# Reordering the opening and the last tiles of a fused linear-attention and two-expert kernel on one core

## The reference

```python
for t in range(S):                                   # attention, per batch and head
    cur = (u * k_t) outer v_t
    y_t = r_t @ (state + cur)
    state = w_t[:, None] * state + k_t outer v_t
x = y, heads side by side                            # 3072 tokens x 384
h = x @ w_in                                         # first expert, 384 -> 1024
solu = h * softmax(h); ln = (solu - mean) / sqrt(var + 1e-6) * g_ln
x = ln @ w_out                                       # 1024 -> 384
h = x @ w_in2; out = maximum(0.01 * h, h) @ w_out2   # second expert, 384 -> 2048 -> 384
```

## Time and profile before

| what | value |
|---|---|
| median of 3 runs | 788.29 us (788.03 to 789.04) |
| the profiled execution's own time | 792.25 us |
| its span, first to last instruction | 790.1 us |
| mean granted TensorE clock | 0.997 of full |
| PE / DVE / ACT / POOL busy | 99 / 66 / 43 / 23% of the span |
| DMA | 45.89 MB, 58 GB/s over the span |

### The profile page before, as it was taken

One profiled execution on the slowest core, in us unless ns is written; L12 is line 12 of the kernel. 1 busy time (PEld: TensorE's weight loads), 2 busy tenths in 40 slices (PEclk: granted clock), 3 DMA queues, 4 the chain that ended last, 5 costly groups with the idle time before them and its releaser, 6 DMA issues.

```text
span 790.1 us, 12141 instructions
## 1 busy us (share of the span) xinstructions
PE 779.6 (99%) x4638; PEld 735.4 (93%) x4638; DVE 517.6 (66%) x1020; ACT 341.5 (43%) x676; POOL 179.5 (23%) x203
## 2 busy tenths in 40 slices
PE   8999999999999999999999999999999999999997
PEld 4779999999999999999999999999999999999997
DVE  7787999966666676657747567485674765553432
ACT  4468554534334353443434443344443434334332
POOL 4751413330222212212212123022120230100000
PEclk9999999999999999999999999999999999999999
DMA  9960122122113021020120310202202111000001
GB/s 256 314 214 6 62 66 66 32 64 66 36 31 96 1 66 44 23 95 6 61 66 1 96 46 21 66 18 79 66 1 66 44 53 31 1 1 31 0 1 35
DMA packets 19666, 45.89 MB, mean 58 GB/s; under 512 B 1952, under 2 KB 14752, under 8 KB 19216
## 3 DMA queue, kind: packets, MB, share of 16 engines
q1 hardware_dynamic: 15952, 37.17, 15.6%
q10 hardware_dynamic: 3648, 7.87, 3.1%
HBM read 40.31 MB, written 4.72 MB: 57 GB/s over the span
## 4 chain that ended last, share of the span: by engine, by line
PE 80%; DVE 1%; issue 0%; ACT 0%; DVEq 0%
PE BANKS L1187 56%; PE MISC L1187 20%; PE BANKS L1366 2%; PE MISC L1211 1%; PE MISC L1204 1%; DVE ki L873 0%; DVE W2L L1021 0%; DVE att L863 0%; DVE A L886 0%; DVE Rraw L1005 0%; DVE RL L1012 0%; DVE X2L L1027 0%; ACT X2H L744 0%; ACT OUT L750 0%; DVE diag L893 0%
## 5 line engine op out<-in xcount | busy, mean ns | idle before, releaser
L1187 PE MATMUL BANKS<-RH,W4H 128*128 128x384 f32 x384 | 135.4, 353 | 0.0
L1187 PE MATMUL BANKS<-X2H,W3H 128*128 128x384 f32 x384 | 130.8, 341 | 0.2 <-DVE X2L L1027 0.2
L1187 PE MATMUL BANKS<-X2L,W3H 128*128 128x384 f32 x384 | 129.4, 337 | 0.0
L1187 PE MATMUL BANKS<-RH,W4L 128*128 128x384 f32 x384 | 129.2, 336 | 0.0
L1187 PE MATMUL BANKS<-X2H,W3L 128*128 128x384 f32 x384 | 129.2, 336 | 0.0
L1187 PE MATMUL BANKS<-RL,W4H 128*128 128x384 f32 x384 | 129.0, 336 | 0.0
L1005 DVE TENSOR_TENSOR Rraw<-BANKS,Rraw 128x384 f32<-128x384 f32 x128 | 70.7, 552 | 86.7 <-ACT Rraw L723 85.7
L723 ACT ACTIVATE Rraw<-BANKS 128x384 f32<-128x384 f32 x128 | 62.6, 489 | 136.5 <-PE BANKS L1187 136.3
L727 ACT ACTIVATE RH<-Rraw 128x384 fp32r<-128x384 f32 x128 | 67.1, 524 | 101.5 <-DVE Rraw L1005 101.5
L873 DVE RECIPROCAL ki<-att 112x128 f32<-112x128 f32 x96 | 89.5, 938 | 0.0
L1012 DVE TENSOR_TENSOR RL<-Rraw,RH 128x384 fp32r<-128x384 f32 x128 | 71.7, 560 | 22.5 <-ACT RH L727 22.5
(11 more groups left out here) (141 smaller groups left out, 1500.7 us busy)
## 6 DMA issues: line engine op xcount, KB each, us to landing
att<-rkw SPq DMA_DIRECT2D x23, 672.0 KB, 4.8
rtok<-r_tok SPq DMA_DIRECT2D x22, 192.0 KB, 2.6
ktok<-k_tok SPq DMA_DIRECT2D x22, 192.0 KB, 2.7
vtok<-v_tok SPq DMA_DIRECT2D x22, 192.0 KB, 3.4
out<-OUT SPq DMA_DIRECT2D x7, 576.0 KB, 4.3
W3raw<-w_in ACTq DMA_DIRECT2D x1, 3072.0 KB, 20.5
W4raw<-w_out ACTq DMA_DIRECT2D x1, 3072.0 KB, 13.5
W1raw<-w_in SPq DMA_DIRECT2D x2, 768.0 KB, 12.1
```

The source lines that it names most:

```text
L1187: return nc.tensor.matmul(dst, lhsT, rhs, start=start, stop=stop, skip_group_check=True)
```

## The change

1. SP: the decays of chunk 1 get a transfer and a semaphore of their own, as chunk 0's have. The order of issue becomes: chunk 0, decays of chunk 1, u, tokens of chunk 0, r and k of chunk 1, then as before. DVE's `decay(0, 1)` waits for the decays alone; `undecayed_keys` and POOL's `decayed_queries` of the first three chunks wait for the rest.
2. POOL: in chunk 0 the own-token products stand ahead of `end_keys`.
3. DVE: `own_sums(0, 0)` stands ahead of the first reciprocal of chunk 1, and `row_max(0, 0)` ahead of the third masks.
4. PE: one `unread` goes; the second half of `first_expert(0)` stands ahead of the scores of chunk 2.
5. PE: the last nine groups of three matmuls go in the order DRAIN, pairs of (output, tile).

```diff
+DRAIN = ((0, 0), (0, 1), (1, 0), (1, 1), (2, 0), (0, 2), (1, 2), (2, 1), (2, 2))
...
+            def load_decay(m):
+                sp.dma_start(att[:, m, 2, :, :].rearrange("p a t -> p (a t)"),
+                             rkw[m * PD:(m + 1) * PD, 2 * PAIRS * CH:3 * PAIRS * CH]).then_inc(ld_decay[m], 16)
...
-                if first(b, m) and m == 0:
-                    sp.dma_start(to[:, 2, :, :].rearrange("p a t -> p (a t)"),
-                                 rkw[0:PD, 2 * PAIRS * CH:3 * PAIRS * CH]).then_inc(ld_decay, 16)
+                if first(b, m) and m < 2:
+                    if m == 0:
+                        load_decay(0)
                     both, part = slice(0, 2), slice(0, 2 * PAIRS * CH)
...
             load_T(0, 0)
+            load_decay(1)
+            sp.dma_start(ub[:, :], u.partition_broadcast(CH)).then_inc(ld_u, 16)
+            load_tok(0, 0)
             load_T(0, 1)
-            load_tok(0, 0)
-            sp.dma_start(ub[:, :], u.partition_broadcast(CH)).then_inc(ld_u, 16)
...
             def decayed_queries(b, m):
+                if first(b, m):
+                    wait_T(pool, b, m)
...
             decayed_queries(0, 0)
-            end_keys(0, 0)
             pool.wait_ge(ld_u, 16)
             own_token(0, 0, 0)
+            end_keys(0, 0)
             own_token(0, 0, 1)
...
             def decay(b, m):
-                if first(b, m) and m == 0:
-                    dve.wait_ge(ld_decay, 16)
+                if first(b, m) and m < 2:
+                    dve.wait_ge(ld_decay[m], 16)
...
             def undecayed_keys(b, m, portion=(0, PAIRS)):
                 a, n = portion
+                if first(b, m):
+                    wait_T(dve, b, m)
...
             mask(0, 0, 2)
-            inverse(0, 1, 0)
             own_sums(0, 0)
-            inverse(0, 1, 1)
+            for a in (0, 1):
+                inverse(0, 1, a)
...
             take_state(0, 1)
+            row_max(0, 0)
             for a in (0, 2):
                 mask(0, 2, a)
             own_sums(0, 2)
-            row_max(0, 0)
...
-            def cons(b, kind, so, f, fp):
+            def cons(b, kind, so, f, fp, outs=range(KM)):
...
-                for m in range(KM):
+                for m in outs:
...
-                last.then_inc(pe_cons, 1)
+                if KM - 1 in outs:
+                    last.then_inc(pe_cons, 1)
...
-                    if len(waiting) > 2:
+                    by_output = closing(b, kind, so) and f == F2 - 1
+                    if len(waiting) > 2 and not by_output:
                         cons(b, *waiting.pop(0))
...
+                    if by_output:
+                        for m, i in DRAIN:
+                            cons(b, *waiting[i], (m,))
+                        waiting = []
...
             first_state(0)
-            unread(1)
             first_transposes(0)
...
             first_state(1)
+            first_expert(0, (1,))
             first_scores(2)
-            first_expert(0, (1,))
             first_transposes(1)
```

More of the change, by code:

```diff
@@ L255, in build @@
         consts, chain = sem("consts"), sem("chain")
-        ld_decay, ld_w1a, filled = sem("ld_decay"), sem("ld_w1a"), sem("filled")
+        ld_decay = [sem("ld_decay0"), sem("ld_decay1")]
+        ld_w1a, filled = sem("ld_w1a"), sem("filled")
         split_hi = [sem(f"split_hi{i}") for i in range(4)]
```

## The result

| | before | changed |
|---|---|---|
| median, 20 runs each | 788.39 us | 791.96 us |
| lowest to highest | 786.46 to 793.44 us | 789.92 to 797.2 us |
| profiled execution, own time / span | 792.25 / 790.1 us | 790.98 / 788.9 us |
| mean granted clock in the profiled one | 0.997 | 1.0 |

The ratio is 1.0036 [1.002, 1.0052]: the changed kernel is slower by about 2.8 us, and the forecast of 787.5 us was wrong. (Ratios compare mean times of runs of one call, a run over 1.5% above the fastest of its kernel left out, so they differ somewhat from what two medians give.) The two profiled executions mislead by themselves: that of the changed kernel is 1.0 us under its own median and one of only three in twenty with a mean clock of 1.0, and that of before is 3.9 over its median. So what follows rests on more than this pair.

A forecast was written before the change was run, and what follows sets the result against it. TensorE was taken as the bound, busy 779.6 of 790.1 us, so gains come only at the ends. Head 0.4 plus tail 0.4 made 0.8 us won: 787.5 us forecast (profiled 791.4), range 785.2 to 790.0.

The forecast's parts named there:

- SP's queue: Load issue order at the start: tokens and u taken to land at 10.4 us, first expert 0.5 us sooner.
- T3: Chunk 3's 672 KB transfer, awaited by DVE's decays: landing taken 0.4 us sooner, at 41.2, so first_out(0) at 48.6.
- With tokens at 11.84: Bad bound in the head: end_keys ends at 15.0, 2.0 after PE wants it; first expert starts 1.0 us later.
- rival (b): Clock falls in a 2.2 to 2.6 us hole before first_out(0), losing 1.7: 790.0, or 789.6 with tail; chance 0.17.
- Case (c): The forecast case: chunk 3's transfer within 0.6 us of before, no clock fall, 786.8 to 788.5 us; chance 0.47.
- The bytes up to there are the same: SP's queue: later loads go out some 0.45 us later with unchanged bytes ahead of them.
- rival (a): Chunk 3's transfer lands by 39.2 us, W3 not later: 2.4 won, 2.8 with tail, 785.5 us; chance 0.36.
- The removed unread pair: PE at 15.10 to 16.15 us, beside take_y: removing it costs and gives nothing more.
- The expert half and row_max: Third scores at full clock, 1.73 us; chunk 1 transposes at 29.5 not 32.74, 3.2 us sooner.
- 0.4 won out of 3.2: Head: of 3.2 us gained by PE, only 0.4 survives the wait for chunk 3's transfer before first_out(0).
- W3 gates X(2): ACT waits for W3, landing at 39.75: X of chunk 2 ready at 41.1, third pass 2.2 us sooner, 1.0 given back.
- Tail: Last nine matmul groups reordered: last-landing store gains 0 to 0.5 us, 0.4 taken; 0.1 at risk.

The follow-up runs named there:

- e15_u_last: Kernel before with chunk 1's decays as their own transfer and tokens ahead of the rest of chunk 1, u still behind it: 788.41 us, ratio 0.9981.
- e5_sp_only: Kernel before with only SP's new order, the split decays and their waits; POOL and DVE keep their orders: 797.69 us, ratio 1.0107.
- e2_queue: Kernel before with SP's new order, split decays, own-token products ahead of end_keys, and own_sums ahead of the reciprocals: 792.59 us, ratio 1.0022.
- e6_pool_only: Kernel before with only own-token products ahead of end_keys and own_sums ahead of the reciprocals, SP as before: 792.87 us, ratio 1.0029.
- e9_changed: The changed kernel, unedited, run once more for a second profile: 792.23 us, ratio 1.0023 to before.
- e4_same: The kernel before, unedited, run again under its own name: 789.03 us, ratio 0.9974.
- e10_w3_later: e7_keys_first with ACT's issue of W3 moved behind take_keys(0, 1): 789.7 us, ratio 0.9994 to before.
- e16_keys_t3_first: e7_keys_first with chunk 3's transfer issued ahead of chunk 4's: 789.16 us, ratio 1.0022 to before.
- e7_keys_first: The changed kernel with end_keys(0, 0) put back ahead of the own-token products: 796.52 us, ratio 1.0091 to before.
- e3_drain: Kernel before with only the last nine groups of matmuls in the order DRAIN: 787.8 us, ratio 0.9964.
- e8_fill_hole: The changed kernel with one and a half unread matmul pairs put ahead of the first key transposes: 797.54 us, ratio 1.0093 to before.
- e12_expert_drain: Kernel before with the first expert's second half ahead of the third scores, row_max first, and DRAIN: 787.66 us, ratio 0.9976.
- e13_t3_first: Kernel before with chunk 3's transfer issued ahead of chunk 4's: 788.27 us, ratio 0.9986.
- e14_best: e12_expert_drain with chunk 3's transfer issued ahead of chunk 4's: 786.57 us, ratio 0.9961 to before.
- e17_pool_fill: e6_pool_only with one and a half unread matmul pairs ahead of the first key transposes: 789.99 us, ratio 1.0025 to before.

## Why the prediction was wrong

In short: two steps on SP's queue and one on POOL failed. The tokens landed later than I took them, the hole that this opened on PE can drop the clock, and the queue falls so far behind that T3 comes late whenever the hole does not. Either way first_out(0) comes late. Two numbers support this. Behind first_out(0) both profiles of the changed kernel take 739.2 us (788.9-49.67 and 790.1-50.86), so what differs between them lies ahead of it. And the changed kernel's three runs at a mean clock of 1.0 have 789.92 to 790.98 us, the fifteen at 0.993 to 0.996 have a median of 792.02: the fall costs some 1.2 us here, and without it the kernel is still 1.5 to 2.6 over before's median.

**SP's queue: "I bound their landing by 9.0 and 11.84 and take the middle, 10.4". This step failed.** POOL's own-token product, which waits for all three tokens, started at 11.37 behind vtok: 1.0 later than forecast. The issues weren't the cause: u's took 0.43 us and not 1.13, so vtok went out at 3.62 and not 4.3. The transfers behind u were slower: vtok landed 7.6 us after its issue. u's early place is the cause: e15_u_last differs from e5_sp_only in it alone, and its vtok takes 4.9 us for 7.8. Why this spread of one row over 128 partitions is slow was not tried.

**POOL: the bound was stated, its consequence was not.** "With tokens at 11.84 ... the first expert starts 1.0 later than before" counted the hole at its own length. The profile of the changed kernel shows that: a hole of 1.79 and the first expert at 17.78, 0.4 later. But the second profile, e2_queue's and e6_pool_only's have the granted clock at 0.50 from 15 us on, after holes of 1.95, 1.58 and 1.31, and in e9_changed it is still 0.50 in the whole window to 25 us. I had named this mechanism, rival (b), with the row that shows it (0.92 us of idling and 0.50 behind it), but I looked for it only at 49 us, and had just made a longer hole among narrow matmuls at 13 us by my own bound. Case (c) then said of late tokens "the T3 gate hides it too". In e9_changed it doesn't: PE is so late that T3 is in time, and PE itself is the bound, at 50.86. Of the changed kernel's 20 runs 15 have a mean granted clock of 0.993 to 0.996, so the falling clock is its rule and the first profile the exception. How much is lost can only be estimated, since both profiles of before are over its median. A run's time is some 2.1 us over its span, and from first_out(0) to the end it is 739.7 us in e4_same (787.3-47.62) and 739.2 in the changed kernel. By this estimate before's median of 788.39 has first_out(0) near 46.6 and the changed kernel's 791.96 near 50.6: 4 us lost in the head, 0.5 won behind it. The medians are 3.6 apart, the means 2.8.

**SP's queue again: "The bytes up to there are the same", so T3 only slides by 0.4. Wrong in size and sign, but masked.** The bytes are the same, the time that they take is not: 4.40 MB by 19 us with u in front, 5.52 with it behind (e5_sp_only, e15_u_last), a backlog that the prediction put at nothing. In e5_sp_only, where no hole delays ACT, T3 takes 17.5 us instead of 13.9. The remedies show that it is W3 and T4 competing with it: W3 later (e10_w3_later, ratio 0.9994) or T3 ahead of T4 (e16_keys_t3_first, 1.0022 and three runs of twelve still at 796 or more) where e7_keys_first has 1.0091. This is the mirror of rival (a), which I had named in one sentence and given no price. Had the head gone as I forecast, this would probably have been the result: e7_keys_first is 4 us slower than the changed kernel. The Trainium skill's page "DMA: Bandwidth & Descriptors", section "Queues, rings and completion order", has a DMA engine turn from one queue to the next only after a whole packet. From this the prediction had drawn that T3's landing might jump by microseconds, and it does: the same T3 takes 10.0 us with W3 later and 17.5 in e7_keys_first, which has W3 in its old place. Whether the packets' alternation is the reason, no run here shows.

**"The removed unread pair ... costs and gives nothing": only while POOL is late.** In three profiles with `end_keys` first it leaves 1.37, 1.72 and 1.48 us of idling ahead of the first transposes (e7, e10, e16), and in e7 and e10 the first expert's six matmuls then took 4.39 and 4.54 us instead of 2.84. In the changed kernel the later key work covers it.

**T3 gates first_out(0) by 7.41 us: right.** From the decays' start to first_out(0), where the decays waited for T3, it is 7.40 in the changed kernel (42.27 to 49.67), e4_same, e3_drain, e5_sp_only and e8_fill_hole, 7.39 in e7_keys_first and 7.41 in e12_expert_drain. With the expert half moved the gate is loose below about 37.3: there PE arrives last, at 45.1.

**The expert half and row_max: right.** 1.89 us for 1.89, and no clock fall at 27 us. 3.2 us were forecast at the transposes and 2.3 came, the difference being the head's own delay (17.78 where 16.85 was forecast: 0.9). "0.4 won out of 3.2" holds for it as long as T3 is late; with T3 in time the same edit is worth the step from e13_t3_first's 788.27 to e14_best's 786.57, 1.7 us with DRAIN in it. But of the 3.2 the 1.7 of clock belonged to the one profile that I summed against. Of the eight profiles that keep the third scores first and have a hole of 0.4 to 0.9 us there, only before's and e13_t3_first's show the fall. Against e4_same's 30.85 the changed kernel's 30.42 is 0.4 sooner, not 2.3.

**W3 gates X(2): right.** 41.71 was its copy and 42.23 the third pass, where 41.1 was forecast; W3 landed 1.2 later than I had it (40.96 for 39.75).

**Tail: 0.4 forecast, 0.6 by the medians of the profiles**, not separable by times. That the store which landed last (4.4 us) would gain fits the profiles: with DRAIN none of ten ends is long.

**Sum.** Head 0.4 won: in fact some 4 lost, by the estimate above. The range's upper end, 790.0, was set by rival (b) at 49 us alone; a second place for the same mechanism, with the 1.0 of the bound and a fall over a few microseconds of narrow matmuls, would have put it beyond 792. A slip besides: in rival (a) half of the 2.8 us gives 786.9, not 786.6; the forecast's own sum doesn't use it.

## What to carry to other kernels

When an unknown landing is bounded from both sides, follow the bad bound to its last consequence: a hole on TensorE among narrow matmuls is to be priced with a possible fall of the clock and not at its length alone. Holes of 0.92 us and more had it here in some executions, and it went with 4.8 us in e6_pool_only and some 1.2 in the changed kernel, where T3's gate hides the rest. Look at several executions before summing against one: the profile of before had both a fallen clock and a late T3, which its repetition lacked. Before moving a transfer forward, list which large loads of another engine's queue are then issued sooner, and which small late loads they get ahead of. When one remedy makes a change worse, look for a second loss that the first one was hiding, and undo both.

## What was unexpected of the hardware

- The clock's fall is a matter of chance at the same instructions: of two profiles of the changed kernel, the hole of 1.79 us was followed by 1.00 throughout and that of 1.95 us by 0.50 until at least 25 us. Of two of the kernel before, each with a hole of 0.92 us at 26 us, one fell to 0.50 and one stayed at 1.00. Of e6_pool_only's twelve runs three have a mean clock of 1.0.
- Unread matmuls put into the hole kept the clock at 1.00 in both profiles that have them (e17_pool_fill, e8_fill_hole), where the matmuls around are the same as without.
- A 192 KB read of one row spread over 128 partitions, put in front of a queue, made the three token loads behind it land at 11.2 us instead of 8.1 (7.6 and 4.9 us from the issue of the last), and left the queue 1.1 MB behind at 19 us, long after it had landed itself.
- T3's landing moves between executions of one kernel: the decays that wait for it started at 41.61 in one profile of the kernel before and at 40.22 in the other.
